# A three-stage kernel (attention, experts, gated product): one pair's score products in one run on the half array, masks of tile 3 first, and the orders of four engines changed to match

## The reference

```python
scores = scale * q @ k.T                       # per head, 576 x 576
cum = cumsum(maximum(s, 0))                    # bias = -(cum_i - cum_j), at most 0
scores = where(causal, -1e9, scores + minimum(bias, 0))
attn = exp(scores - max); attn /= sum(attn) + 1e-9
x = (attn @ v), heads side by side             # 1152 x 512
x = experts(x)       # 8 experts of 512-1024-512, weighted by a Sinkhorn-normalised gate
out = ((x @ w_a) * (x @ w_b)) @ w_out          # 512-1536-512
```

## Time and profile before

| what | value |
|---|---|
| time, median of 3 runs | 1083.09 us (1083.08 to 1084.53) |
| the profiled execution | 1083.52 us, of which the span 1081.7 us |
| PE busy | 1072.5 us (99%) |
| PEld, DVE, ACT, POOL busy | 966.4, 704.7, 425.4, 334.2 us |
| granted clock of TensorE | 1.000 (2.4 GHz) |
| chain that ended last | PE 95%; DVE, SP's queue, POOL, issue 1% each |
| starts of the periods k = 0 to 7 | 9.17, 14.34, 27.15, 38.63, 50.09, 61.56, 73.03, 84.52 us |
| end of period 7 | 96.00 us |

### The profile page before, as it was taken

The page is one execution under the profiler, slowest core; times in us unless marked ns, Lnnn a source line. Parts: engine busy times, 40 slices in busy tenths (PEclk is TensorE's granted clock), DMA queues, the critical chain, the costliest instruction groups (busy, mean ns, idle before and its releaser), DMA issues.

```text
span 1081.7 us, 19242 instructions
## 1 busy us (share of the span) xinstructions
PE 1072.5 (99%) x6746; PEld 966.4 (89%) x6746; DVE 704.7 (65%) x1498; ACT 425.4 (39%) x984; POOL 334.2 (31%) x440
## 2 busy tenths in 40 slices
PE   8999999999999999999999999999999999999999
PEld 6777989889898998989899898989989899898997
DVE  7778966666565665647566564756657687486682
ACT  6888637233251523416142341514324433132230
POOL 1445604122140412314042240413214275144420
PEclk9999999999999999999999999999999999999999
DMA  8762211111111111111111111110211102102002
GB/s 185 200 136 71 59 40 40 59 35 45 59 39 39 39 58 39 47 50 39 39 39 58 39 58 39 39 45 33 59 53 45 38 3 79 40 21 76 23 1 88
DMA packets 91702, 59.27 MB, mean 55 GB/s; under 512 B 32736, under 2 KB 78048, under 8 KB 91648
## 3 DMA queue, kind: packets, MB, share of 16 engines
q1 hardware_dynamic: 90448, 58.27, 19.2%
q10 hardware_dynamic: 1200, 0.30, 0.1%
HBM read 56.15 MB, written 2.40 MB: 54 GB/s over the span
## 4 chain that ended last, share of the span: by engine, by line
PE 95%; DVE 1%; SPq 1%; POOL 1%; issue 1%; DMA 0%; ACT 0%; DVEq 0%; POOLq 0%
PE bank L1767 15%; PE bank L1769 14%; PE bank L1768 14%; PE bank L1892 14%; PE bank L1893 14%; PE bank L1894 14%; PE bank L1752 2%; PE bank L1715 2%; PE bank L1646 1%; DVE kept_c L1253 1%; SPq L503 0%; PE bank L1604 0%; PE bank L1686 0%; DMA nat<-in_k 0%; PE bank L1789 0%
## 5 line engine op out<-in xcount | busy, mean ns | idle before, releaser
L694 POOL TENSOR_TENSOR hl<-kept_c,hh 128x320 fp32r<-128x320 f32 (+1 forms) x128 | 104.9, 820 | 525.0 <-ACT kept_c L892 525.0
L1892 PE MATMUL bank<-w2h,hh 128*128 128x512 f32 x680 | 266.2, 392 | 0.0
L1893 PE MATMUL bank<-w2l,hh 128*128 128x512 f32 x680 | 264.8, 389 | 0.0
L1894 PE MATMUL bank<-w2h,hl 128*128 128x512 f32 x680 | 264.8, 389 | 0.0
L1419 DVE SCALAR_TENSOR_TENSOR acc<-bank,P,acc 128x512 f32<-128x512 f32 x135 | 101.4, 751 | 196.0 <-PE bank L1894 196.0
L1767 PE MATMUL bank<-xh,w1h 128*128 128x320 f32 (+1 forms) x704 | 209.7, 298 | 0.4 <-DVE kept_c L1253 0.3
L1253 DVE TENSOR_TENSOR kept_c<-bank,kept_c 128x256 f32<-128x256 f32 (+1 forms) x440 | 183.9, 453 | 38.3 <-PE bank L1769 34.9
L1769 PE MATMUL bank<-xh,w1l 128*128 128x320 f32 (+1 forms) x704 | 208.3, 296 | 0.0
L1768 PE MATMUL bank<-xl,w1h 128*128 128x320 f32 (+1 forms) x704 | 208.3, 296 | 0.0
L890 ACT ACTIVATE hh<-kept_c 128x256 fp32r<-128x256 f32 (+1 forms) x256 | 113.3, 443 | 155.7 <-DVE kept_c L1253 155.7
L791 ACT ACTIVATE kept_one<-bank 128x256 f32<-128x256 f32 (+1 forms) x88 | 34.8, 396 | 322.6 <-PE bank L1769 322.5
(11 more groups left out here) (155 smaller groups left out, 1412.8 us busy)
## 6 DMA issues: line engine op xcount, KB each, us to landing
raw<-in_moe_w SPq DMA_DIRECT2D x32, 512.0 KB, 3.6
raw<-in_moe_w SPq DMA_DIRECT2D x32, 256.0 KB, 2.7
raw<-in_moe_w SPq DMA_DIRECT2D x64, 128.0 KB, 2.7
bias<-cum_dram SPq DMA_DIRECT2D x14, 256.0 KB, 3.5
raw<-in_moe_w_a SPq DMA_DIRECT2D x12, 256.0 KB, 2.9
raw<-in_moe_w_b SPq DMA_DIRECT2D x24, 128.0 KB, 2.9
raw<-in_moe_w_out SPq DMA_DIRECT2D x6, 512.0 KB, 3.7
bias_tail<-cum_dram SPq DMA_DIRECT2D x16, 144.0 KB, 4.3
```

Of the source, the lines that this page charges most:

```text
L694: pool.tensor_tensor(hl[:, 3 - place, columns(b, s)], src[:, 0:width(s)], hh[:, place, columns(b, s)].bitcast(F32), ALU.subtract).then_inc ...
L1892: pe.matmul(bank, hh[:, place, at], w2h[:, place, :], start=(nth == 0), stop=False)
L1893: pe.matmul(bank, hh[:, place, at], w2l[:, place, :], start=False, stop=False)
L1894: ins = pe.matmul(bank, hl[:, 3 - place, at], w2h[:, place, :], start=False, stop=(nth == 3))
```

## The change

```diff
-    BIASED_NTH = {(0, 1): 1, (0, 0): 2, (1, 1): 3, (1, 0): 4, (2, 0): 5, (2, 1): 6, (3, 1): 7, (3, 0): 8}
-    EXP_NTH = {(0, 0): 1, (1, 0): 2, (2, 0): 3, (1, 1): 4, (0, 1): 5, (3, 1): 6, (3, 0): 7, (2, 1): 8}
+    BIASED_NTH = {(2, 0): 1, (2, 1): 2, (0, 1): 3, (0, 0): 4, (1, 1): 5, (1, 0): 6, (3, 1): 9, (3, 0): 10}
+    SCORES_NTH = {2: 1, 0: 2, 3: 5}
+    EXP_NTH = {(2, 0): 1, (0, 0): 2, (1, 0): 3, (1, 1): 4, (0, 1): 5, (3, 1): 6, (3, 0): 7, (2, 1): 8}
...
-            pool.wait_ge(x_hi, 2 * p + g + 1)
             cols = slice(p * S + lo, p * S + hi)
+            if p < PAIRS - 2:
+                pool.wait_ge(x_scaled, 2 * p + g + 1)
+                pool.tensor_copy(xh[:, cols], xr[:, cols]).then_inc(x_first_hi, 1)
+                pool.wait_ge(x_first_hi, 2 * p + g + 1)
+            else:
+                pool.wait_ge(x_hi, g + 1)
...
             copy_pT(k - 1, 7)
-            exp_tile(k, 0, 0)
             high_qk(k + 1, 0)
             copy_pT(k - 1, 1)
-            high_x(k - 2, 0)
             high_qk(k + 1, 1)
             if k == -1:
                 first_bias_rows()
-            exp_tile(k, 1, 0)
-            high_x(k - 2, 1)
+            exp_tile(k, 2, 0)
             copy_pT(k - 1, 6)
             copy_pT(k - 1, 0)
-            exp_tile(k, 2, 0)
+            exp_tile(k, 0, 0)
+            exp_tile(k, 1, 0)
             copy_spread(k - 1, 0)
...
         for k in range(-1, PAIRS):
             scale_x(k - 2, 0)
+            scale_x(k - 2, 1)
             low_qk(k, 2)
-            scale_x(k - 2, 1)
             copy_pT(k - 1, 5)
+            biased(k, 2, 0)
+            biased(k, 2, 1)
+            add_eps(k - 1)
             biased(k, 0, 1)
             biased(k, 0, 0)
-            add_eps(k - 1)
             biased(k, 1, 1)
-            biased(k, 1, 0)
-            biased(k, 2, 0)
             copy_pT(k - 1, 4)
-            biased(k, 2, 1)
             invert(k - 1)
             copy_pT(k - 1, 3)
+            biased(k, 1, 0)
             low_qk(k + 1, 0)
             low_qk(k + 1, 1)
...
+            biased_tail(k, 0)
+            biased_tail(k, 1)
             biased(k, 3, 1)
             biased(k, 3, 0)
-            biased_tail(k, 0)
-            biased_tail(k, 1)
...
+        def masks_ahead(p):
+            pe.wait_ge(sc_done, 10 * p + 6)
+            for r in range(2):
+                pe.matmul(S_BANK[r][:, (FULL - 1) * PART:MAIN], identb[:, :], maskb[:, :], start=True, stop=False,
+                          skip_group_check=True)
...
-                at_least(pe, sc_done, 10 * (p - 1) + 8)
+                at_least(pe, sc_done, 10 * (p - 1) + 10)
...
-                at_least(pe, sc_done, 10 * (p - 1) + 10)
+                pe.wait_ge(tr_lo, 3 * p + 2)
+                at_least(pe, sc_done, 10 * (p - 1) + 8)
...
-                pe.wait_ge(sc_done, 10 * p + 4)
                 score_products(p, 2)
```

More of the change, by code:

```diff
@@ L252, in attention_experts_product @@
     pv_mm = [sem(f"pv_mm{g}") for g in range(2)]
+    x_first_hi = sem("x_first_hi")
     x_hi = sem("x_hi")
@@ L809, in exp_tile @@
             act.wait_ge(sc_done, 10 * p + BIASED_NTH[t, r])
-            if (t, r) == (0, 0):
+            if (t, r) == (2, 0):
                 at_least(act, eps_done, p - 1)
@@ L820, in exp_tail @@
             c = TAIL_COLUMN
-            act.wait_ge(sc_done, 10 * p + 10)
+            act.wait_ge(sc_done, 10 * p + 8)
             tile = scores_tail[z][:, 0:S]
@@ L1160, in biased @@
             col = PART if t == 1 else 0
-            if (t, r) in ((0, 1), (2, 0), (3, 1)):
-                dve.wait_ge(sc_mm, 5 * p + max(t, 1))
+            if (t, r) in ((2, 0), (0, 1), (3, 1)):
+                dve.wait_ge(sc_mm, 5 * p + SCORES_NTH[t])
             if p == 0:
                 dve.wait_ge(first_bias, r + 1)
-            elif (t, r) == (0, 1):
+            elif (t, r) == (2, 0):
                 at_least(dve, pt_mm, 8 * (p - 1))
@@ L1176, in biased_tail @@
             first = neg_max[:, z, TAIL_FIRST:TAIL_FIRST + 1]
-            dve.wait_ge(sc_mm, 5 * p + 4 + half)
+            dve.wait_ge(sc_mm, 5 * p + 3 + half)
             if half == 1:
-                dve.wait_ge(sc_done, 10 * p + 9)
+                dve.wait_ge(sc_done, 10 * p + 7)
             elif p == 0:
@@ L1364, in _ @@
             cols = slice(last * S + lo, last * S + hi)
-            dve.wait_ge(x_hi, 2 * last + s + 1)
+            dve.wait_ge(x_hi, 2 + s + 1)
             dve.wait_ge(x_lo, 2 * last)
@@ L1645, in score_products @@
                         rows = slice(r * D, (r + 1) * D)
-                        pe.matmul(S_BANK[first + r][:, col:col + n], qk[z][rows, a, 0, t * PART:(t + 1) * PART],
-                                  qk[z][rows, b, 1, 0:n], start=(nth == 0 and i == 0), stop=False)
+                        if g < 2:
+                            pe.matmul(S_BANK[first + r][:, col:col + n], qk[z][rows, a, 0, t * PART:(t + 1) * PART],
+                                      qk[z][rows, b, 1, 0:n], start=(nth == 0 and i == 0), stop=False)
+                        else:
+                            ins = pe.matmul(S_BANK[first + r][:, col:col + n],
+                                            qk[z][rows, a, 0, t * PART:(t + 1) * PART], qk[z][rows, b, 1, 0:n],
+                                            start=False, stop=(i == 2), skip_group_check=True)
+            if g == 2:
+                ins.then_inc(sc_mm, 1)
+        def masks_ahead(p):
+            if not present(p):
+                return
+            pe.wait_ge(sc_done, 10 * p + 6)
+            for r in range(2):
+                pe.matmul(S_BANK[r][:, (FULL - 1) * PART:MAIN], identb[:, :], maskb[:, :], start=True, stop=False,
+                          skip_group_check=True)
         def score_masks(p, g):
@@ L1794, in _ @@
             transpose_qk(k, 2)
-            score(k, 0)
+            for g in (0, 1) if k == 0 else (1, 0):
+                score(k, g)
             transpose_p(k - 1, 5)
+            score_masks(k, 1)
+            transpose_p(k - 1, 2)
             score_masks(k, 0)
-            transpose_p(k - 1, 2)
-            score(k, 1)
+            transpose_qk(k + 1, 0)
             transpose_p(k - 1, 7)
[L1801 to L1804, removed]
             transpose_qk(k + 1, 1)
@@ L1807, in _ @@
                 spread_first_bias()
-            score(k, 2)
+            transpose_p(k - 1, 1)
+            score_tail(k, 0)
+            transpose_p(k - 1, 4)
             transpose_p(k - 1, 3)
-            score_masks(k, 2)
+            score_tail(k, 1)
             transpose_p(k - 1, 6)
-            score_tail(k, 0)
             transpose_p(k - 1, 0)
-            score_tail(k, 1)
+            masks_ahead(k)
             spread_recips(k - 1, 1)
             spread_recips(k - 1, 0)
+            score(k, 2)
+            attend(k - 1, 0)
             attend(k - 1, 1)
-            attend(k - 1, 0)
         def make_first(p, n, sem, value):
```

## The result

The changed kernel takes 1087.12 us, the median of 10 runs (1086.13 to 1088.58), against 1084.26 for the kernel before on the same chip (10 runs, 1082.95 to 1085.98): a ratio of 1.0025, 95% interval 1.0016 to 1.0034. Slower, inside the range, by 2.9 us where +4.5 was forecast. That the forecast of 1087.6 lies only 0.5 from the result is in part luck: it was built on 1083.09, the median of 3 runs of the kernel before, and ten runs put that kernel at 1084.26, 1.2 higher. The profiled execution took 1087.10 with a span of 1085.3.

The account below looks back on a forecast made before the run. TensorE was taken as the bound, with its own list plus seams. Periods 0 and 1 +1.6, five steady periods +2.35, period 7 +0.55: +4.5 us, 1087.6 us; own range 1085.2 to 1089.4, 8 in 10 1083.2 to 1089.8.

Parts of the forecast that it names:

- TensorE's list, 10.98 us: TensorE's own work in a steady period, forecast to shrink by 0.49 us to 10.98 as seams go.
- The S1 seam: Entry and exit cost of score products S1 among full-array transposes; removing it gives back 0.34 us a period.
- The seam S2|A0: Where S2 now meets attend, both using half the array differently: still charged; if free, 0.15 us a period more.
- The ring: Groups T4, T6, spread1 wait for copies out of reused banks: 0.94 us stall, net +0.47 a steady period.
- the walk: Adding matmul, copy and signal times from T4 to spread1: 2.92 us needed against 1.98 of TensorE's work.
- Periods 0 and 1: Start of the kernel: QK1 of period 1 meets the load of k at 20.06, period 2 starts 1.6 us later.
- Period 7: Last period: +0.2 us from the ring and 0.35 from GpSimd's stretched L637, together +0.55.
- At nothing: Parts forecast to cost nothing: the cast `high_x` moved to GpSimd, tile 3's exponentials, VectorE's steps, transfers, what follows the loop.
- rival 3: Another engine is late: tile 3's exponentials or `scale_x(1)` make TensorE wait 0.4 us each period; 1090.4 us; chance 10%.
- Rival 1: Copies before T6 and spread1 stay hidden: 0.49 us gained in 7 periods, faster at 1079.7 us; chance 13%.
- Rival 2: A draw: short signals, free seam S2|A0, QK1's load in time; +0.7 to +2 us, 1084.5; chance 13%.
- Rival 4: Seams do not go: drain paid per switch of head, 0.49 us gain missing, stall stays; 1091 us; chance 2%.

Follow-up runs that it names:

- the sixth: Kernel before, with S1 moved directly behind QK2 and S0, S2 and the other engines' orders unchanged: 1082.79 us, ratio 0.9986.
- the fourth experiment: Changed kernel with the copies of T4 and T6 cut to a quarter, TensorE's instructions the same: 1083.93 us, ratio 0.9997.
- the first experiment: Changed kernel with S2 moved from behind the two spreads to directly ahead of them: 1084.88 us, ratio 1.0007.
- the control with short copies: Kernel before, with the copies of T4 and T6 cut to a quarter from the second pair on: ratio 0.9988.
- the tenth experiment: The sixth, with VectorE's two 576 wide differences moved behind its steps of tile 3: 1081.88 us, ratio 0.9981.
- the seventh: Changed kernel with the cast `high_x` back on ScalarE, where it was before: 1087.05 us, ratio 1.0026.
- the second experiment: Changed kernel with QK1 moved between T3 and T6 and tail1 between T6 and T0: 1089.69 us, ratio 1.0045.
- the third: The second experiment with ScalarE's copies of T6 and T0 ahead of QK1's high part, VectorE's QK1 low part behind the tails: 1087.17 us, ratio 1.0026.
- the ninth experiment: Changed kernel with VectorE's two 576 wide differences of period 7 moved behind the tail's biased scores: 1086.46 us, ratio 1.0025.
- the fifth's with T4's copy: Changed kernel with only VectorE's copy of T4 cut to a quarter from the second pair on: 1085.64 us, single run.

## Why the prediction was right, and where its sizes were off

- **TensorE's list, 10.98 us.** Right. The S1 seam gave 0.34 where it was removed alone (the sixth), and the change with short copies leaves 10.99.
- **The seam S2|A0 is paid.** Right: S2 to attend is 73.11 - 72.22 = 0.89, what S2 to T3 took before, and attend's weight load stands 1.8 / 5 = 0.36 us, twice the 0.18 of the seam that the prediction took as its nearest. The Trainium skill (TensorEngine Tiling (Array Packing), Key Properties) has a drain at a change of tiling mode; by that rule this seam costs, and the trace agrees.
- **The ring, +0.47 a period.** Right in mechanism, and over by 0.18: +0.29. The places are the ones named (T6 and spread1, with T0 and the masks between them). Of the prediction's signs, the view of waits shows ScalarE ahead of the spread; T6's wait for VectorE, 0.1 us, is too short to be listed there. What was mis-sized is the term "from the end of a result to the waiting matmul I take 0.145". Measured it is 0.05 behind T4's copy and 0.04 behind T6's, which alone makes 2.92 into 2.73, the low end of 0.75 that the prediction had kept. The 0.145 came from two waits of other kinds. One is score products behind a `biased` step, and the two waits of that kind in the change's period 1 took 0.15 again (though the masks ahead started 0.06 behind such a step). The other is the spread behind GpSimd, whose release was as slow again in the fourth experiment (68.23 to 68.37).
- **What the walk left out.** It took the small stalls on VectorE as lying "inside" ScalarE's. In length they do, but they are a second chain, not slack: without ScalarE's wait 0.38 of 0.75 us stayed (the first experiment). No single cover that was tried repaired the change.
- **Periods 0 and 1, +1.6.** Mis-sized: +0.8 at full clock. The step that failed is "There it meets the load of k ... so QK1 stays at 20.06". The load isn't a fixed wall, though it was issued at 14.4 us in all of these programs. It released QK1 at 20.06, at 19.92 in the control with short copies, at 20.14 in the tenth experiment and 19.47 in the first; but QK1 ran at 18.98, 19.11 and 19.20 without waiting for it in the sixth, the fourth (the change with short copies) and the seventh. So what differs is the landing; why it does was not tried. With the load in time, the front is late only by VectorE's ten steps, as the walk up to T5 had it (17.6; the seventh has 17.5).
- **Period 7, +0.55.** +0.38, the same two parts: L642 stretched by 0.57 (0.35 was taken, of 0 to 1.0), and part of this lay beside the ring's wait.
- **At nothing.** Right for the cast (the seventh). TensorE's waits show nothing for tile 3's exponentials, `scale_x` or `bd` in the steady periods, so rival 3 didn't come. Rival 1 needed a stall under 0.49; it was 0.78. Rival 2, the draw, had half of the truth: short signals and the load in time, but not the free seam. Rival 4 fell with the sixth experiment.
- **The range.** Its own bounds, added up, give about +1.75 to +5.8 (0.9 or 1.6, five times 0.13 or 0.6, and 0.2 or 1.2), not +2.1 to +6.3. The +2.9 lies inside either.

Each of the two seams was worth what its rows said. What made the change a loss, with the 1.2 us of periods 0, 1 and 7, is that it takes the fillers, QK1 and S2, from between the units whose copies the ring waits for. Removing the S1 seam without touching T4 to spread1 keeps the gain.

## What to carry to other kernels

Where groups take turns on a few banks, walk the ring with the copies' times before an order is changed to please TensorE: the work between a group and the one that reuses its bank must last as long as its matmuls, the copy and the signal, and a gain on the list counts only while this holds at every place. When cover is moved, move the copying engine's order with it (the second experiment against the third), and look for the second chain that ends just before the first: undoing one alone gives the difference between them. Price a signal from the same kind of wait: the same two engines, and the same kind of group that waits.

## What the runs showed that was not expected

- A transpose behind a copy of ScalarE or VectorE started 0.04 to 0.05 us after the copy's end; behind GpSimd's reciprocals it was 0.14 (68.23 to 68.37).
- GpSimd's 64 wide scalar product takes 0.44 us by itself, 1.01 in the change's period 7 and 1.54 beside VectorE's two 576 wide differences; a cast of 320 went from 0.45 to 0.98 (the ninth experiment).
- The same load, issued by the same queue at 14.4 us, was in by 18.98 us in the sixth experiment's execution and released its waiter at 20.14 in the tenth's.
- Executions of one kernel differ by single stretches of 3.4 us at the 1.2 GHz level. In the change's profiled execution one lay in periods 0 and 1, with TensorE busy all through the 3.3 us ahead of it, and these periods took 0.5 us more (19.30 against 18.79). In five of the others (the fourth experiment and its control, the fifth's with T4's copy, the seventh, the tenth) it began 882 to 886 us into the span, shortly behind an idle stretch of TensorE of 1.9 us; the executions whose clock stayed full there have the same idle stretch. In the seventh the time from QK2 of period 7 to the end was 998.4 us with it, and 997.6 in the change without. That is a fair part of the 2.9 us that were to be measured.
